# Tile 2's turn-over at an earlier slot, and another order of the operand splits and weight loads

## The reference, cut to what matters

```python
keep = is_sink | in_window          # pos < 4, or 0 <= query - key < 128
scores = np.where(keep, scale * q @ k.T, -1e9)
a = np.exp(scores - max); a = a / (sum(a) + 1e-9)
x = (a @ v), heads side by side                       # 1536 x 512
h = np.maximum(x @ w_in, 0); x = (h * h) @ w_out      # layer 1
h = x @ w_in2                                         # layer 2
g = (a0 + a1 h + a2 h^2 + a3 h^3) / (1 + |b0||h| + |b1| h^2 + 1e-6)
out = g @ w_out2
```

## Time and profile before

| what | value |
|---|---|
| median of 3 runs | 652.62 us (651.33 to 652.8) |
| the profiled execution's own time | 652.8 us |
| its span, first to last instruction | 651.0 us |
| PE busy, PE weight loads busy | 640.4 us (98%), 598.1 us (92%) |
| DVE, ACT, POOL busy | 451.9, 391.5, 281.8 us |
| chain that ended last | PE 85%, DVE 10%, POOL 2% |

### The profile page before, as it was taken

The page is one execution under the profiler, slowest core; times in us unless marked ns, Lnnn a source line. Parts: engine busy times, 40 slices in busy tenths (PEclk is TensorE's granted clock), DMA queues, the critical chain, the costliest instruction groups (busy, mean ns, idle before and its releaser), DMA issues.

```text
span 651.0 us, 10444 instructions
## 1 busy us (share of the span) xinstructions
PE 640.4 (98%) x3792; PEld 598.1 (92%) x3792; DVE 451.9 (69%) x694; ACT 391.5 (60%) x867; POOL 281.8 (43%) x314
## 2 busy tenths in 40 slices
PE   8999999999999999999999989999999999999997
PEld 6879999999999999999999979888999999999995
DVE  5755556355655545443577789999898889998995
ACT  4655766356555555443322277778777787778774
POOL 2799554000000000000122258777777777777773
PEclk9999999999999999999999999999999999999999
DMA  7766411061111321000334310011100210001001
GB/s 244 217 221 232 140 41 41 1 203 42 40 41 42 107 73 49 10 1 1 98 129 129 119 46 1 1 38 60 50 0 1 98 49 2 0 1 50 1 1 53
DMA packets 28971, 43.49 MB, mean 67 GB/s; under 512 B 4080, under 2 KB 19440, under 8 KB 28400
## 3 DMA queue, kind: packets, MB, share of 16 engines
q1 hardware_dynamic: 28912, 42.74, 19.9%
HBM read 36.44 MB, written 6.29 MB: 66 GB/s over the span
## 4 chain that ended last, share of the span: by engine, by line
PE 85%; DVE 10%; POOL 2%; ACT 1%; issue 1%; DVEq 0%; ACTq 0%; POOLq 0%
PE h_ps L1312 25%; PE y_ps L1324 21%; PE y_ps L1602 15%; PE s_ps L1312 7%; PE o_ps L1312 4%; DVE s_ps L997 3%; PE o_ps L1422 3%; PE s_ps L1366 2%; PE s_ps L1379 2%; DVE o_ps L997 2%; DVE p_buf L1000 2%; DVE p_buf L991 1%; DVE h_ps L997 1%; PE s_ps L1362 1%; PE o_ps L1431 1%
## 5 line engine op out<-in xcount | busy, mean ns | idle before, releaser
L1312 PE MATMUL h_ps<-xT,weights 128*128 128x384 f32 x960 | 189.3, 339 | 0.3 <-DVE sq L1007 0.3
L1312 PEld LDWEIGHTS h_ps<-xT,weights 128*128 128x128 f32 x960 | 167.4, 188 | 4.0 <-issue 2.7
L1324 PE MATMUL y_ps<-hid,weights 128*128 128x384 f32 x768 | 154.5, 341 | 0.0
L1602 PE MATMUL y_ps<-weights,hid 128*128 128x512 f32 x576 | 144.3, 395 | 2.4 <-POOL hid L609 1.0
L518 POOL TENSOR_SCALAR weights<-weights_raw 128x1024 fp32r<-128x1024 f32 x24 | 25.3, 1053 | 266.3 <-DMA weights_raw<-in_w_pack 266.3
L1324 PEld LDWEIGHTS y_ps<-hid,weights 128*128 128x128 f32 x768 | 133.7, 188 | 1.1 <-issue 1.1
L1602 PEld LDWEIGHTS y_ps<-weights,hid 128*128 128x128 f32 x576 | 107.2, 188 | 24.3 <-POOL hid L609 2.4
L692 ACT ACTIVATE sq<-sq 128x384 f32<-128x384 f32 x64 | 33.5, 524 | 115.3 <-DVE sq L1007 115.3
L609 POOL TENSOR_TENSOR hid<-p_buf,hid 128x384 fp32r<-128x384 f32 x63 | 64.8, 1029 | 39.9 <-ACT hid L877 39.6
L997 DVE RECIPROCAL s_ps<-q_buf 128x384 f32<-128x384 f32 x31 | 79.4, 2561 | 3.2
L600 POOL TENSOR_TENSOR q_buf<-h_abs,q_buf 128x384 f32<-128x384 f32 x64 | 64.9, 1015 | 34.5 <-ACT q_buf L665 32.1
(11 more groups left out here) (121 smaller groups left out, 835.5 us busy)
## 6 DMA issues: line engine op xcount, KB each, us to landing
weights_raw<-in_w_pack SPq DMA_DIRECT2D x32, 512.0 KB, 3.8
bk_raw<-in_k_pack SPq DMA_DIRECT2D x24, 256.0 KB, 3.4
q_pair<-in_q_pack SPq DMA_DIRECT2D x21, 256.0 KB, 3.3
bv<-in_v_pack SPq DMA_DIRECT2D x24, 128.0 KB, 2.2
y_scratch<-xT SPq DMA_DIRECT2D x2, 1536.0 KB, 6.1
xT<-y_scratch SPq DMA_DIRECT2D x2, 1536.0 KB, 6.5
out_y<-out_stage SPq DMA_DIRECT2D x3, 768.0 KB, 3.5
inv_cols<-in_q_pack SPq DMA_DIRECT2D x3, 256.0 KB, 3.6
```

What stands on the lines that cost most here:

```text
L1312: ins = nc.tensor.matmul(bank, weights[:, i, wp, W_IN, t * P:(t + 1) * P], x, start=(t == 0 and n == 0), stop=(t == KC - 1 and n == 2))
L1324: ins = nc.tensor.matmul(y_ps[:, m, 0:NT], weights[:, i, wp, W_OUT, m * P:(m + 1) * P], hid[:, i % 2, gp, :], start=(i == 0 and n == 0), s ...
L1602: ins = nc.tensor.matmul(y_bank(turn, t), hid2[:, i % RING, gp, t * P:(t + 1) * P], weights[:, i, wp, W_OUT, :], start=(i == 0 and n == 0) ...
```

## The change: one slot, one queue order and two interleavings

Four edits, all on the banded path:

1. `slots_before(2)` is 27 instead of 28 (the other two stay 12 and 20), and ACT and DVE take `done_at` too, so that `tile_out(2)` stands after slot 27 on all three engines; `split_at` is gone.
2. SP: w8 and w9 are no longer loaded ahead of k = 10. The triples move: w8 to w10 behind the keys and queries of k = 10, w11 to w13 behind those of k = 11, w14 and w15 behind those of k = 12.
3. POOL: w5 is made ahead of the splits, w6 between `split_earlier(8)` and `split_kq(8)`, w7 between `split_earlier(9)` and `split_kq(9)`. Before, the order was w0 to w4, `split_earlier(8)`, `split_earlier(9)`, `split_kq(8)`, `split_kq(9)`, w5, w6, w7.
4. ACT: the high parts of w8 to w15 are made at the ends of i = 1 to 8 instead of i = 2 to 9.

```diff
         def slots_before(qt):
-            return H * qt + H + 4
+            return H * qt + (H + 4 if qt < 2 else H + 3)
...
-        def split_at(s):
-            return [qt for qt in range(QT) if (slots_before(qt) if qt + 1 < QT else LEAD - 1) == s]
...
-                load_weights(0, EARLY)
-                load_weights(0, EARLY + 1)
                 for k in range(EARLY + 2, GROUPS + 1):
                     if k < GROUPS:
                         load_k(k)
                         load_q(k)
-                    for i in range(3 * k - 20, min(3 * k - 17, FT)):
+                    for i in range(3 * k - 22, min(3 * k - 19, FT)):
                         load_weights(0, i)
...
-                for i in range(5):
+                for i in range(6):
                     weight_high(0, i)
                     weight_low(i, w_high, i + 1)
                 pool.wait_ge(ks_loaded, 16)
-                for split in (split_earlier, split_kq):
-                    for k in (EARLY, EARLY + 1):
-                        split(k)
-                for i in range(5, EARLY_W):
-                    weight_high(0, i)
-                    weight_low(i, w_high, i + 1)
+                split_earlier(EARLY)
+                weight_high(0, 6)
+                weight_low(6, w_high, 7)
+                split_kq(EARLY)
+                split_earlier(EARLY + 1)
+                weight_high(0, 7)
+                weight_low(7, w_high, 8)
+                split_kq(EARLY + 1)
...   (on ACT and on DVE, in the lead)
-                    for qt in split_at(s):
+                    for qt in done_at(s):
                         tile_out(qt)
...   (on ACT)
-                        if blk == 0 and 2 <= i < FT - EARLY_W + 2:
-                            weight_high(i + EARLY_W - 2)
+                        if blk == 0 and 0 < i <= FT - EARLY_W:
+                            weight_high(i + EARLY_W - 1)
```

## The result

Seven timed runs of the changed kernel have a median of 656.19 us (655.13 to 657.87), seven of the kernel before 652.57 us. The ratio is 1.0059, 95% interval 1.0043 to 1.0076: 3.6 us by the medians, slower. The forecast was 655.2 us with 652.8 to 657.2; the time lies in the range, 1.0 us above the forecast. The profiled execution took 656.43 us, its span is 654.6 us.

What follows compares the result with a forecast made beforehand. PE was taken as the bound, busy 640.4 of 651.0 us. The greater delay, POOL's 2.5 us over the turn-over's 1.7, made 652.8 + 2.5 = 655.3; with the runs' median 0.2 us below the profiled one, 655.2 us was predicted, range 652.8 to 657.2.

Steps and rivals of the forecast that it cites:

- The turn-over: Tile 2's turn-over after slot 27 delays ACT's copy of unit 27, so PE starts unit 30 1.7 us later.
- POOL's order: w5 and w6 ahead of the end of split_kq(8) make PE start unit 32 2.5 us later (2.1 to 3.0).
- The greater of the two, not the sum: At unit 32 the 1.7 us and 2.5 us delays do not add up; the shift behind it is 2.5 us.
- w6 to be made at 3.88 or 4.25 us: POOL's time for w6 ahead of split_kq(8); the slower if VectorE's subtraction holds POOL up, making the sum 2.6 us.
- The moved loads hidden, with a cover of 0.0 to 0.8 us: w8 lands at 58.9 to 59.8; ACT waits up to 0.8 us, but PE's unit 34 loses nothing.
- the rival to which I gave 0.14: w8 lands later than 59.8 and ACT's wait reaches PE at unit 34; 656.3 to 657.3 us, chance 0.14.
- The clock: Rival: PE's clock falls to 1.2 GHz behind the pause of about 2.0 us ahead of unit 30; 656.5 us, chance 0.06.
- The sum: Whole kernel: 652.8 us of the profiled execution + 2.5 = 655.3, with 655.2 us predicted.
- its own list of signs: Signs expected in the changed profile, among them POOL's wait for w5, PE's at unit 32 and unit 34 at about 61.5.
- PE's start of the second layer: Sign behind unit 32: the prediction is wrong if this start moves by another amount than unit 32 has.
- the loads' term: The moved weight loads, w8 landing 4.0 to 4.9 us after issue at 54.9, were to cost PE nothing at unit 34.

Runs made afterwards that it cites:

- e2_pool: The kernel before with POOL's new order alone (w5 to w7 among the splits); 657.33 us, ratio 1.0082.
- e4_tile_back: The changed kernel with the turn-over of tile 2 back at slots 28 and 29; 657.40 us, ratio 1.0081.
- e5_act_back: The changed kernel with ACT's copies of the weights one i later, as before; 655.59 us, ratio 1.0054.
- e10_fill_both: The changed kernel with three idle matmuls in PE's pause ahead of unit 30 and two ahead of unit 32; 655.54 us, ratio 1.0047.
- e1_tile: The kernel before with the turn-over of tile 2 alone moved to slot 27; 653.62 us, ratio 1.0023.
- e8_w8_alone: The changed kernel with w9 and w10 loaded ahead of the keys and queries of k = 10, w8 still behind them; 655.44 us, ratio 1.0052.

## Why the prediction was right, and where it was short

- *The turn-over*, 1.7 us at unit 30: right to 0.1 us in the changed kernel's profile. PE's pause there is 2.12 us (forecast about 2), and DVE's low part is at 38.53, with the 1.1 us of the start 39.6 as worked out. The other profiles give a little less: from the scores of unit 27 to unit 30 it is 5.27 to 5.54 us in the six with the turn-over moved and no filling, 3.68 to 4.04 in the five without the move, 1.5 us between the means.
- *POOL's order*, 2.5 us (2.1 to 3.0) at unit 32: right in kind, short in size. It is 3.2 us in the changed kernel, and a pause of 3.25 instead of 0 in e2_pool. That is above the upper bound, so this term was mis-sized, though its wait is the one forecast. From POOL's start on w5 to unit 32 it is 16.1 to 16.5 us in all eight profiles with the new order, where the sum has 15.7. Two terms were too small. w5 lands 0.2 to 0.3 us later than in the one row (4.9 instead of 4.6 us from its issue), and `split_kq(8)` takes 4.94 us (48.18 to 53.12) where I took the 4.25 of the earlier trace rows and a little more: its first operation has 0.94 us instead of 0.62, and ahead of `bq_lo` POOL stands for 0.51 us, where it was 0.14. All profiles with the new order have these 0.51 us; why is open. The row of the other split, 4.7 us, was nearer.
- *The greater of the two, not the sum*: shown by the waits of e4_tile_back.
- *w6 to be made at 3.88 or 4.25 us*: it took 3.90 here and in e5_act_back, and 4.22 to 4.29 in the other six profiles with the new order. What the Trainium skill (GPSIMD Engine Reference, Specifications) says of the interfaces that POOL shares with VectorE agrees with these traces: what POOL does beside VectorE's subtraction of a hidden tile, which has two inputs in SBUF, is mostly 0.3 to 0.4 us longer, or the subtraction is (1.05 and 1.14 us in the changed kernel, 0.56 to 0.60 in e10_fill_both). In the six that subtraction falls inside w6. In the changed kernel it starts at 47.51 and reaches into the split's first operation, the 0.94 us above. The prediction counted this cost once at most, for w6, and not again inside the split. Its sum with a slow w6 comes to 2.5 us, not 2.6.
- *The moved loads hidden, with a cover of 0.0 to 0.8 us*: this step failed; the rival to which I gave 0.14 came in. I took w8's landing at 4.0 to 4.9 us. It was 6.4 us, and PE lost another 1.4 us at unit 34. The 4.0 us is the row of w13, like w8 the first of three behind keys and queries, and it is the fastest such landing in any profile; the 4.9 us is that of a weight issued alone. The first of the triple issued at 44.51 before took 6.7 us, with other loads around it. It should have been the upper bound: 54.9 + 6.7 gives 61.6 and a wait at unit 34. Why the same kind of load takes 4.0 us in one place and 6.4 in another is open.
- *The clock*: 0.06 was too low. In the changed kernel three of eight executions have a mean clock of 0.996 or 0.997 and a median of 656.86 us, the five others 655.33. That the clock fell in these three is concluded from the mean; none of them has a trace, and the profiled one has 1.00 behind both pauses. The forecast missed it in its sum, though not in its list. The lower level could be seen in the profile before, at its end, behind PE's last work.
- *The sum*: that the number is only 1.0 us off is in part luck. By the rows the loss up to unit 34 is 4.6 us where I forecast 2.5, and the difference of the spans is smaller only because PE's start in the changed kernel's profile was 1.1 us earlier. I did not know of that scatter of the start, and a forecast made against one execution carries it. The five executions with a mean clock of 0.998 or more have a median 2.8 us over before, less than these rows give, so the wait at unit 34 may be shorter or absent in some of them; no trace shows it. (The median of before is 0.2 us under the profiled execution, so 655.3 should have become 655.1.)

By its own list of signs the prediction failed in one: PE's start of the second layer was to move by the same amount as unit 32. With the 1.1 us, unit 32 moved by 3.2 us and all behind unit 34 by 4.5 to 4.6.

The size of the loads' term is what separates forecast and rival: with w8 landing after 6.4 us the same working has ACT free of `inv_copy(3)` at 54.9 + 6.4 + 1.04 + 0.60 = 62.9, PE at unit 34 at 63.0 instead of 59.04, and 656.8 us.

## What to carry to other kernels

Read each in-order engine's program as a queue: an edit that is harmless for the unit it serves holds up all that is behind it, here the copies of units 28 and 27 and the split of unit 32. Delays on several side engines count at the point where the bound engine meets them, and the latest counts, not the sum; but one long pause of PE can cost more than two short ones of the same sum, since the clock may fall behind it. When a load is moved behind a wait, bound its landing by the slowest of the loads issued like it, not by the fastest row.

## What the runs showed of the hardware that was not expected

- Behind a pause of PE of 3.25 us the granted clock fell to 0.50 in the profile of POOL's order alone, and behind one of 2.1 us in that of the turn-over alone, within about 2 us of PE's return; it was back at 1.00 some 3 to 4 us later. Each fall that nothing covered cost 1.5 us. With the pause of 2.1 us alone, 1 of 8 executions has a mean clock under 0.998; with one of over 3 us all ten of e2_pool and e4_tile_back. The length of the pause does not decide by itself: the same pause of 2.1 us ahead of unit 30 brought the low clock in two of six profiles (e1_tile and e8_w8_alone), and one of 2.40 us at unit 32 of e8_w8_alone did not. The Trainium skill (TensorE: Matmul & The Clock Gate, Why this matters for your kernels) advises against long pauses between bursts of matmuls for this reason; the traces agree that they lower the clock.
- The very first matmuls of the kernel take between 4.42 and 5.49 us in profiled executions of the same instructions, and the rows behind them are that much earlier or later, 1.1 us. The granted clock shown is 1.00 in both. By the scores of unit 27 the profiles stand up to 1.6 us apart (34.74 to 36.38), so this start is not the only source.
- Three 512 KB loads issued together landed 6.4, 7.2 and 7.9 us after their issue in the changed kernel. The first of such three took 4.0 to 8.4 us over all profiles, one alone 4.2 to 5.6 and once 6.9.
- Beside VectorE's subtraction with two inputs in SBUF, GpSimd's operations mostly took 0.3 to 0.4 us longer, as 0.94 instead of 0.62 us, or the subtraction itself took about 1.1 instead of 0.6.
